# Attention block with a low-rank token mixing: the mixing in 64x128 tiles of TensorE, A and V in plain f32, the softmax denominators behind the turned weights

## The reference, cut to what matters

```
scores = q @ k.T / 8 + bias        # band of 96 positions and 8 global ones; 2 batches, 8 heads, 768 positions
a      = softmax(scores)           # a = exp / (sum + 1e-9)
x      = a @ v                     # (batch, 768, 512)
h      = x.transpose(0, 2, 1) @ U @ V        # U 768x32, V 32x768: the mixing over positions
u      = x + h.transpose(0, 2, 1)
y      = u + relu(u @ w_ch1) @ w_ch2         # 512 -> 2048 -> 512
xk, xr = mixtures of y and of y one position before
out    = sigmoid(xr @ w_r) * (relu(xk @ w_k) ** 2 @ w_v)
```

## Time and profile before

| what | value |
|---|---|
| time, median of 3 runs | 524.44 us (520.75 to 524.69) |
| time of the profiled execution | 523.01 us |
| its span | 521.3 us |
| PE busy | 508.3 us (98%) |
| PEld busy | 423.4 us (81%) |
| DVE, ACT, POOL busy | 183.7, 130.9, 243.1 us |
| attention and seven mixings | from 0 to 90.94 us |
| channel stages | from there to the end |

### The profile page before, as it was taken

One profiled execution on the slowest core, in us unless ns is written; L12 is line 12 of the kernel. 1 busy time (PEld: TensorE's weight loads), 2 busy tenths in 40 slices (PEclk: granted clock), 3 DMA queues, 4 the chain that ended last, 5 costly groups with the idle time before them and its releaser, 6 DMA issues.

```text
span 521.3 us, 10020 instructions
## 1 busy us (share of the span) xinstructions
PE 508.3 (98%) x3968; PEld 423.4 (81%) x3968; DVE 183.7 (35%) x479; ACT 130.9 (25%) x352; POOL 243.1 (47%) x228
## 2 busy tenths in 40 slices
PE   4999999999999999999999999999999999999997
PEld 3888887888888888888888888888888888888885
DVE  5677776121313313133131331312443233441323
ACT  3787885101100011100111001121322132203220
POOL 3255557166007200079700729990899579960000
PEclk9999999999999999999999999999999999999999
DMA  6876764204001200014400000000000200020002
GB/s 204 273 248 204 238 203 172 84 1 160 1 0 59 104 0 0 0 61 150 162 29 0 0 1 0 1 0 0 1 0 1 81 0 0 0 80 0 0 0 80
DMA packets 15347, 33.88 MB, mean 65 GB/s; under 512 B 1489, under 2 KB 1873, under 8 KB 15313
## 3 DMA queue, kind: packets, MB, share of 16 engines
q1 hardware_dynamic: 14736, 32.57, 18.6%
q10 hardware_dynamic: 576, 0.84, 0.5%
HBM read 30.25 MB, written 3.15 MB: 64 GB/s over the span
## 4 chain that ended last, share of the span: by engine, by line
PE 93%; DVE 4%; ACT 1%; DMA 1%; issue 1%; POOL 0%; ACTq 0%; POOLq 0%
PE psum L587 25%; PE psum L575 25%; PE psum L631 13%; PE psum L640 13%; PE psum L655 6%; PE psum L430 4%; DVE probs L868 2%; PE psum L468 2%; PE psum L444 1%; PE psum L483 1%; PE psum L486 1%; ACT probs L686 1%; PE psum L460 1%; DMA k_in<-in_k 1%; PE psum L484 1%
## 5 line engine op out<-in xcount | busy, mean ns | idle before, releaser
L983 DVE SCALAR_TENSOR_TENSOR HL<-psum,HH 128x512 fp32r<-128x512 f32 x48 | 33.2, 692 | 171.8 <-ACT HH L767 171.8
L767 ACT ACTIVATE HH<-psum 128x512 fp32r<-128x512 f32 x48 | 28.7, 599 | 229.2 <-PE psum L575 229.2
L587 PE MATMUL psum<-HH,w2h 128*128 128x512 f32 x192 | 75.1, 391 | 0.0
L575 PE MATMUL psum<-UH,w1h 128*128 (+1 forms) x192 | 74.9, 390 | 0.0
L587 PE MATMUL psum<-HL,w2h 128*128 128x512 f32 x192 | 74.8, 390 | 0.0
L575 PE MATMUL psum<-UH,w1l 128*128 (+1 forms) x192 | 74.8, 390 | 0.0
L587 PE MATMUL psum<-HH,w2l 128*128 128x512 f32 x192 | 74.8, 389 | 0.0
L575 PE MATMUL psum<-UL,w1h 128*128 (+1 forms) x192 | 74.8, 389 | 0.0
L1105 POOL TENSOR_SCALAR w1h<-raw 128x2048 fp32r<-128x2048 f32 x4 | 7.7, 1922 | 118.0 <-PE psum L587 118.0
L686 ACT ACTIVATE probs<-probs,neg_max 128x192 f32<-128x192 f32 x96 | 42.5, 444 | 21.0 <-DVE neg_max L868 20.5
L1022 DVE TENSOR_TENSOR k_square<-k_relu 128x512 f32<-128x512 f32 x24 | 24.0, 1001 | 66.5 <-ACT k_relu L792 66.4
(11 more groups left out here) (118 smaller groups left out, 880.4 us busy)
## 6 DMA issues: line engine op xcount, KB each, us to landing
v_in<-in_v SPq DMA_DIRECT2D x16, 384.0 KB, 4.0
raw<-in_moe_w_ch SPq DMA_DIRECT2D x6, 1024.0 KB, 5.2
v_rest<-in_v_rest SPq DMA_DIRECT2D x8, 384.0 KB, 3.7
out<-result SPq DMA_DIRECT2D x12, 256.0 KB, 2.0
k_in<-in_k SPq DMA_DIRECT2D x7, 432.0 KB, 4.4
q_in<-in_q SPq DMA_DIRECT2D x7, 384.0 KB, 3.5
raw<-in_moe_w_ch SPq DMA_DIRECT2D x8, 256.0 KB, 3.9
raw<-in_moe_w_v SPq DMA_DIRECT2D x2, 1024.0 KB, 5.1
```

The source lines that it names most:

```text
L575: mm = pe.matmul(bank[4 + f % 2][:, 0:BLK], w[:, kt, f * P:(f + 1) * P], x[:, kt, ds(blk * BLK, BLK)], start=kt == 0 and n == 0, stop=kt = ...
L587: mm = pe.matmul(bank[d][:, 0:BLK], w[:, f, d * P:(d + 1) * P], x[:, f % 2, :], start=f == 0 and n == 0, stop=f == FQ - 1 and n == 2)
L767: act.activation(HH[:, f % 2, :], bank[4 + f % 2][:, 0:BLK], ACT.Relu).then_inc(hid_high, 1)
L983: dve.scalar_tensor_tensor(out=HL[:, f % 2, :], in0=bank[4 + f % 2][:, 0:BLK], scalar=0.0, in1=HH[:, f % 2, :].bitcast(F32), op0=ALU.max, ...
```

## The change

x is transposed in halves of 64 positions, one half of each tile to bank 6 and the other to bank 7, in tiles of 64x128, the form of `turn`. A and V stay in plain f32: rows 0 to 63 of `A4` (blocks 0 and 1, which is all of A) multiply the first 64 positions of every tile, rows 64 to 127 (the same again) the others, each in one f32 matmul of 192 columns, added to the transposes. The rounding of V on POOL and `a_low` on DVE go, and with them `v_split`, `a_high` and `v_rows`. ACT's copy of A is plain f32 and releases PE itself. The copy to `Y` reads both banks. Bank 6 held the denominators; these move to the last columns of bank 2, which `turn` fills, so DVE waits for `turn(n-2)` first, computes the denominators of unit n-3 and then evacuates.

```diff
-        VH4 = region("VH4", [P, S], F32R)
-        VL4 = region("VL4", [P, S], F32R)
-        A4 = region("A4", [P, 2, P], F32R)
+        V4 = region("V4", [P, S])
+        A4 = region("A4", [P, 2, P])
...
-        denom = psum[:, 6, 0:4]
-        M_BANK = 7
+        denom = psum[:, TURN_BANKS[0], 2 * WIN:2 * WIN + 4]
+        dense_denom = psum[:, 6, 0:1]
+        MIX_BANKS = (6, 7)
+        MIXED = psum[:, 6:8, 0:HALF // GROUPS]
...
             def mixed(x, slot, half):
-                to = bank[M_BANK]
-                cols = slice(half * HALF, (half + 1) * HALF)
-                pe.matmul(to[:, 0:HALF], A4[:, slot, :], VH4[:, cols], start=True, stop=False)
-                pe.matmul(to[:, 0:HALF], A4[:, slot, :], VL4[:, cols], start=False, stop=False)
+                tokens = V4[:, half * HALF:(half + 1) * HALF].rearrange("r (i j c) -> r j i c", j=GROUPS, c=GROUP)
                 for i in range(ST // 2):
-                    mm = pe.matmul(to[:, i * P:(i + 1) * P], x(half * ST // 2 + i), ident[:, :],
-                                   is_transpose=True, start=False, stop=i == ST // 2 - 1)
+                    for j in range(GROUPS):
+                        q = group(j)
+                        pe.matmul(bank[MIX_BANKS[j]][:, i * GROUP:(i + 1) * GROUP], x(half * ST // 2 + i)[q],
+                                  ident[q, j * GROUP:(j + 1) * GROUP], is_transpose=True, start=i == 0, stop=False)
+                for j in range(GROUPS):
+                    mm = pe.matmul(bank[MIX_BANKS[j]][:, 0:HALF // GROUPS].rearrange("p (i c) -> p i c", c=GROUP),
+                                   A4[group(j), slot, :], tokens[group(j), j], start=False, stop=True)
                 mm.then_inc(mix_done, 1)
...
-                    act.activation(A4[:, p % 2, :], bank[M_BANK][:, 0:P], ACT.Copy).then_inc(a_high, 1)
+                    act.activation(A4[:, p % 2, :], bank[MIX_BANKS[0]][:, 0:P], ACT.Copy).then_inc(a_ready, 1)
...
-                act.activation(y_slice(p, part - 1), bank[M_BANK][:, 0:HALF], ACT.Copy).then_inc(y_kept, 1)
+                act.activation(y_slice(p, part - 1).rearrange("p (i j c) -> p i j c", j=GROUPS, c=GROUP),
+                               MIXED.rearrange("p j (i c) -> p i j c", c=GROUP), ACT.Copy).then_inc(y_kept, 1)
...
-            def a_low(p):
-                dve.wait_ge(a_high, p + 1)
-                r = slice(2 * RANK, 4 * RANK)
-                dve.tensor_tensor(A4[r, p % 2, :], bank[M_BANK][r, 0:P], A4[r, p % 2, :].bitcast(F32),
-                                  ALU.subtract).then_inc(a_ready, 1)
-
             def banded_attention():
                 for n in range(NU + 3):
+                    if 2 <= n < NU + 2:
+                        dve.wait_ge(pt_done, 2 * (n - 2) + 2)
+                    if n >= 3:
+                        denominators(n - 3)
                     if 2 <= n < NU + 2:
                         evac(n - 2)
                     if n < NU:
                         maxima(n)
                     if n == 0:
                         even_tiles()
-                    if piece(n) and piece(n)[1] == 0:
-                        a_low(piece(n)[0])
                     if n >= 3:
                         normalise(n - 3)
...
-            def factors():
-                pool.wait_ge(uv_in, 32)
-                pool.tensor_scalar(VH4[:, :], v_rows[:, :], 1.0, 1.0, ALU.mult, ALU.mult).then_inc(v_split, 1)
-                pool.wait_ge(v_split, 1)
-                pool.tensor_tensor(VL4[:, :], v_rows[:, :], VH4[:, :].bitcast(F32), ALU.subtract).then_inc(v_split, 1)
```

More of the change, by code:

```diff
@@ L158, in block_kernel @@
         end = region.at
-        region = Region(y_at + 2 * 4 * KT * TOK - 4096)
-        v_rows = region("v_rows", [P, S])
         region = Region(y_at)
@@ L217, in block_kernel @@
         uv_in = sem("uv_in")
-        v_split = sem("v_split")
         bounds_set = sem("bounds_set")
@@ L244, in block_kernel @@
         a_done = sem("a_done")
-        a_high = sem("a_high")
         a_ready = sem("a_ready")
@@ L397, in _ @@
                     sp.dma_start(U[:, :, :], mix_u).then_inc(uv_in, 16)
-                    sp.dma_start(v_rows[:, :], mix_v).then_inc(uv_in, 16)
+                    sp.dma_start(V4[:, :], mix_v).then_inc(uv_in, 16)
                     sp.dma_start(mu[:, :, :], mus).then_inc(mu_in, 16)
@@ L475, in sums_of_x @@
                     for side in (t % 2, t % 2 + 2):
-                        mm = pe.matmul(bank[M_BANK][side * RANK:(side + 1) * RANK, 0:P], U[:, t, :], x(t),
+                        mm = pe.matmul(bank[MIX_BANKS[0]][side * RANK:(side + 1) * RANK, 0:P], U[:, t, :], x(t),
                                        start=t < 2, stop=t >= ST - 2)
@@ L501, in mixing @@
                     pe.wait_ge(a_ready, p + 1)
-                    pe.wait_ge(v_split, 2)
                 else:
@@ L563, in _ @@
                 pe.wait_ge(uv_in, 32)
[L564 to L568, removed]
+                for p in range(PAIRS - 1):
+                    dense_mixing(p, p % 2)
             def hidden(Q, blk, f, w1h, w1l):
@@ L874, in evac @@
             def evac(n):
-                dve.wait_ge(pt_done, 2 * n + 2)
                 if n >= 2:
@@ L878, in evac, with denominators @@
                 dve.tensor_copy(probs_t[:, n % 2, 0, :], bank[TURN_BANKS[0]][:, 0:2 * WIN]).then_inc(ptevac[0], 1)
-            def normalise(n):
-                p, u = n // UNITS, n % UNITS
+            def denominators(n):
                 dve.wait_ge(exp_done, 2 * n + 2)
@@ L887, in normalise @@
                 dve.wait_ge(norm_step, 2 * n + 2)
+            def normalise(n):
+                p, u = n // UNITS, n % UNITS
                 dve.wait_ge(pv_done, n + 1)
@@ L969, in _ @@
                         dve.wait_ge(baton, tile_step(h, t, 20))
-                        dve.tensor_scalar(denom[:, 0:1], bank[4][:, D:D + 1], 1e-9, None, ALU.add).then_inc(baton, 1)
+                        dve.tensor_scalar(dense_denom, bank[4][:, D:D + 1], 1e-9, None, ALU.add).then_inc(baton, 1)
                         dve.wait_ge(baton, tile_step(h, t, 21))
-                        dve.reciprocal(inv_denom[:, 0:1], denom[:, 0:1]).then_inc(baton, 1)
+                        dve.reciprocal(inv_denom[:, 0:1], dense_denom).then_inc(baton, 1)
                         dve.wait_ge(baton, tile_step(h, t, 22))
@@ L977, in _ @@
                 dve.sem_inc(norm_done, NU)
-                for p in range(PAIRS - 1):
-                    a_low(p)
             def low_half(step, f):
@@ L995, in _ @@
             low_half(0, 1)
-            a_low(PAIRS - 1)
             low_half(0, 2)
@@ L1117, in _ @@
                 prepare_pair(1)
-                factors()
                 for p in range(PAIRS):
```

## The result

| | before | with the change |
|---|---|---|
| median, all runs of the comparison | 524.1 us (520.75 to 524.69, 6 runs) | 528.96 us (526.16 to 531.03, 6 runs) |
| profiled execution | 523.01 us | 526.16 us |
| its span | 521.3 us | 524.4 us |

The ratio is 1.0101, with a 95% interval from 1.0061 to 1.014: slower by about 1%, where I forecast 520.5 us. The time lies above my range. In the experiments, executions that are over 1.5% longer than the fastest of the same kernel, at a lower granted clock, are left out of the medians: two of experiment 9 (530.97 and 534.31 us), one of 10 (538.12) and two of 11 (534.12 and 536.17).

The account below looks back on a forecast made before the run. PE was taken as the bound, busy 508.3 of 521.3 us. Terms -2.6 - 0.7 - 0.5 + 0.4 = -3.4 gave 519.6 us from the profiled 523.01, 521.0 from the median; forecast 520.5 between them, range 516.8 to 524.6.

Parts of the forecast that it names:

- The hand-over: From attention to channel stages: PE starts L575 earlier until held by POOL's last weight piece, -0.5 us.
- my -2.6 us for the mixings: Mixings on PE before the channel stages: 11 x 0.24 us saved, -2.6 us (-2.1 to -3.1).
- A `mixed`: Net cost of one mixing on PE: 0.55 us against 0.79, with six transposes at 0.21 and the product at 0.34.
- rival 1: Mixing products overlap only by half: three passes, 0.51 us, `mixed` at 0.72; 521.8 us from the profiled time; chance 0.17.
- 3: Rival: tiles don't work side by side in the mixing product, 0.68 us, `mixed` at 0.89; 524.2 us; chance 0.05.
- 4: Rival: weight loads show in the mixing product, 1.23 us, `mixed` at 1.44; 533 us; chance 0.04.
- The wait for A: PE's wait for ACT's copy of A in the attention's first mixings disappears: 5 x 0.14 = -0.7 us.
- Three turns: PE in the attention, from one `turn` to the third after it: 9.1 us instead of 9.69.
- Denominators on DVE, ACT and POOL's rounding at nothing: DVE's new order, ACT's copies and POOL's lost rounding of V were each costed at nothing.
- The tail: Pair 7's mixing among the channel stages' 128x128 tiles: 0.88 us instead of 0.68, +0.2 us twice, +0.4 us.
- rival 2: Deeper gain: transposes at 0.17, A waits gone in all seven pairs, POOL's chain shorter: -4.9, 518.1 us; chance 0.17.
- if L569 starts as soon as PE gets there: Sign of failure at the first channel matmul; the forecast had PE idle there until POOL's piece releases it.

Follow-up runs that it names:

- experiment 9: Changed kernel, one looped copy of the path not taken, q, k, v loads spread, 36 identity transposes ahead of the first scores: 524.98 us, ratio 1.0033.
- 10: Kernel before the change, with spread loads and 36 identity transposes ahead of the first scores: 532.22 us, ratio 1.0147.
- 11: Kernel before the change, with only 36 identity transposes added ahead of the first scores, loads as before: 526.09 and 526.58 us.
- experiment 6: Changed kernel, one looped copy of the path not taken, 16 of 128 rows of q, k, v loaded from pair 2 on: 517.05 us, ratio 0.9876.
- experiment 3: Changed kernel with the path not taken as the old loop and DVE's old order, denominators in SBUF: 527.55 us, ratio 1.0109.
- 7: Kernel before the change, with 16 of 128 rows of q, k and v loaded from pair 2 on: 521.07 us, ratio 0.9956.
- experiment 5: Changed kernel with the path not taken as one copy of the mixing in a loop of seven: 523.94 us, ratio 1.0013.
- 1: Changed kernel with the path not taken as the old loop again, three copies of the mixing instead of seven: 528.05 us, ratio 1.0098.
- experiment 2: Kernel before the change, with only its path not taken unrolled on PE as in the change: 530.21 us, ratio 1.014.
- 4: Changed kernel with 16 of 128 rows of v loaded from pair 2 on: 524.65 us, ratio 1.0037.
- 13: Changed kernel, one looped copy of the path not taken, PE waiting for the second channel weights only before their first matmul: 522.61 us, ratio 1.0004.
- experiment 8: Changed kernel, one looped copy of the path not taken, loads spread (k at a pair's start, q a turn later, v two): 525.58 us, ratio 1.0045.

## Why the prediction was wrong

The failed step is the hand-over, -0.5 us, with its sentence that what is late next is POOL's piece, and the cost of nothing that I gave PE's own program everywhere. I costed the second path at nothing, without a word, because its instructions are not run. I forecast L569 4 to 4.5 us earlier than 90.94, released by POOL; it came at 92.01, 2.7 us behind POOL's piece and 2.6 us behind the packet, after 4.55 us of gaps that my -2.6 us for the mixings had no place for. What the change removes and adds in the mixing I had nearly right.

Point by point:

- **A `mixed`, 0.55 us forecast:** 0.47 measured. The six transposes take 0.18 (I took 0.21), the product 0.48 less the 0.19 that a change of shape costs anyway (0.61 - 0.42), so 0.29 (I took 0.34). The tiles run side by side; rivals 1, 3 and 4 are out. The rule of the Trainium skill, TensorE: Matmul & The Clock Gate, Part 3 (The mechanism), that matmuls start and end strictly in program order, read as in rival 1, would have made the product three passes, 0.51: the trace disagrees here too.
- **The wait for A:** gone; L440 to L481 is 0.42 to 0.43 where the earlier trace rows have 0.66.
- **Three turns, 9.1 us forecast:** 8.92 without a gap, and 8.91 in experiment 6, from 44.55 to 53.46 on its timeline; with the gaps in them 10.27 (from 56.66 to 66.93).
- **Denominators on DVE, ACT and POOL's rounding at nothing:** right. By experiment 3 their new place costs nothing that can be seen (there they also lie in SBUF instead of PSUM).
- **The hand-over, POOL's piece late next:** right where nothing else is in the way (experiment 6, 0.59 us of wait). Up to there the gain is 4.16 us by experiments 6 and 7, I had 2.6 + 0.7 + 0.5 = 3.8. In the changed kernel the fetch is later than POOL and hides it.
- **The tail, +0.2 us twice:** 0.91 against 0.68. Right. From the start of the channel stages to the end experiment 6 takes 515.1 - 84.30 = 430.8 us, experiment 7 518.8 - 88.46 = 430.3.
- **The sum, -3.4 us:** -4.0 by the medians of experiments 6 and 7, between my sum and rival 2's -4.9. Had the program been there in time, this is what the change gives.

What ate it, in the two profiled executions. The channel stages begin 92.01 - 90.94 = 1.07 us later. That is -4.2 (the mixing and its waits), -1.8 (the first `sums_of_x` starts at 24.41 instead of 26.18, because the full clock came sooner; in ten other executions, of either mixing, it starts between 24.49 and 25.53, so this is taken as the execution's, not the change's), +4.2 (gaps inside: 4.55 less the 0.38 of before), and +2.9 (the jump): +1.1. Behind it 432.39 us against 430.36, +2.0: eight matmuls at half the pace, 8 x 0.20 = 1.6, and the tail's 0.4. Together +3.1, the difference of the spans.

That the granted clock is full all through, as I wrote of the kernel before, isn't so. Its windows read 1.00 from the start, but up to 21 us its turns run at half the pace, as in this row, where the change's L426 already takes 0.98 us at 18.53:

```profile
19.02 1.72 PE L430 MATMUL psum<-k_in,q_in 64*64 64x160 f32 x32
```

The median of the change lies 2.8 us above this execution, the fastest of its six. The three at a mean granted clock of 0.989 (0.996 here) took 528.66 to 531.03 us. More half clock behind gaps inside the attention, as in experiment 5, would do that; there is no trace of them, so it isn't shown.

By experiments 5 and 1 the shorter path gave back 4.1 us of medians, and by 6 against 5 the loads account for 6.9, of which the kernel before has 2.0 itself.

Two signs I had and passed over. The list of waits of before has two gaps of 0.2 us by "issue" in the attention; they stand three blocks of the program apart, to two records. And the diff shows plainly that a loop becomes seven copies. My sign of failure, "if L569 starts as soon as PE gets there", asked for the wrong thing as well: it started later than both PE and POOL.

## What to carry to other kernels

Cost the program as you cost the data: an edit that adds instructions to an engine near its bound, or speeds up the work between them, needs 16 KB of program sooner, while the data queues are full. Code that is jumped over is not free: keep it short, a loop instead of copies, and look at the trace even so (experiment 9). If an idle stretch reads "issue" in the midst of one operation's records, count the records to the next one and look at when the instruction queue's packet came.

## What the runs showed of the hardware that I had not expected

- From an instruction packet to the first instruction behind it: 2.2 to 2.5 us inside the attention, 2.5 to 2.9 at the jump (packets at 89.4, 92.4, 95.2, 97.5, 89.6 and 90.4; starts at 92.01, 95.19, 97.68, 100.22, 92.45 and 93.17).
- In experiments 2 and 10 some 3 us more pass between PE's arrival and the packet (92.2 to 95.2, 94.4 to 97.5), in experiments 1 and 11 and in the change 0.3 at most. I can't say what fills them; nothing was tried on it.
- 72 instructions of no use ahead of all work bring a gap of 3.16 us and eight matmuls at half pace into the kernel before (526.09 and 526.58 us against a median of 523.05), and with a shorter path not taken the gap at the jump is gone (524.11).
- A gap can cost twice: at the jump in the change 2.9 us of idleness and 1.6 us of half clock behind it, in experiment 2 5.49 us and eight matmuls at 0.43. Behind gaps of 1.5 us the granted clock fell in experiments 4 and 13 and stayed in the change; behind 1.27 at the jump of experiment 9 it stayed.
- What stays open: why a packet comes late. It is late in stretches of a DMA share near 1, and small loads take the gaps away, which shows that the loads bring most of them; by which queue or engine of the transfers it is held up, the runs don't tell, and spreading the loads (experiment 8) didn't help.
